# Routing of a mixture-of-experts kernel rewritten: constants ahead of attention, flags on GpSimd, 16-bit one-hot tables, expert 0's weights in batches 1 and 2

## The chip, the cores and the metric

The kernel is one program on one core of a Trainium2 chip. The metric is its device time in microseconds (us), as the median of several executions. The profile and the trace describe one execution. Engines: PE is TensorE, DVE is VectorE, ACT is ScalarE, POOL is GpSimd, SP is SyncE, which here only issues transfers (DMAs).

## The reference

Three stages run one after the other, on 4 batches of 576 positions and 512 channels (8 heads of 64), all in float32:

```python
# 1. windowed attention: heads 0-3 see the last 32 positions, heads 4-7 every 4th of the last 128
attn = softmax(where(mask, q @ k.T / 8, -1e9)) ; x = attn @ v          # (4, 576, 512)
# 2. mixture of 8 experts, one expert for each token
for b in range(B):
    prev_e = -1
    for s in range(S):
        fresh_e = argmax(x[b, s] @ w_gate)
        e = fresh_e if s == 0 or sigmoid(x[b, s] @ w_local) < 0.5 else prev_e
        prev_e = e
        out[b, s] = softmax(x[b, s] @ w_gate)[e] * (relu(x[b, s] @ w1[e]) @ w2[e])
# 3. gated convolution: sigmoid(5-tap causal conv of out) * (out @ w_val), then @ w_out
```

The choice of an expert runs along the sequence: a token either takes its own best expert or keeps the one of the token before it.

## The kernel before, in words

**Attention.** 48 steps (`STEPS` = 12 for each batch: 4 pairs of heads, 3 groups of 2 tiles of 96 queries). In step `s` PE makes the scores of step s, the transposes of s-1, the products with v of s-2 and so on; DVE masks and takes the maximum of s (`mask_and_max`), divides s-2 by its denominator into `x_plain` or `x_dil` (`norm`), and adds up the 9 gate logits of s-5 (`take_logits`). SP's queue, written out by hand, loads `qT`, `kT` and `vwin` ahead of their steps, stores the attention output to `x_tokens` in DRAM, and takes the logits of the dilated heads through DRAM (`dil_logits`, then `lg_back`) to bring them back into token order. Three waits on DVE depend on SP's stores: `norm` of the first step of a batch waits until `x_dil` of the batch before is in DRAM (`dil_stored`), `norm` of its seventh step the same for `x_plain`, and the last `take_logits` of a batch waits for `lg_back` (`lg_loaded`). In the schedule `norm(36)`, the first of batch 3, and the sum of batch 2's logits both stand in the steps that follow step 36.

**Expert weights.** Each expert has four chunks of 128 x 2048. A chunk is loaded twice: by POOL's DMA into `w_high` with rounding (`load_high`), and by SP's into `stage` (`load_raw`, two buffers). POOL then subtracts one from the other into `w_low` (`split`, L564), because every product is made as three passes of rounded parts (`passes`, L1159).

**Routing** is what stands between attention and the first expert tile. DVE takes the largest logit, the best expert, the keep flag (`keep`), and its complement (`anew`). PE transposes `keep` and `start` so that the 96 tokens of a tile lie along a row, DVE scans each row, the ends of the 24 rows are transposed and scanned (`carry`), and the carried choice goes back to [96, 24] (`choice`). `chosen` holds for each token a one-hot row over the experts. Two matmuls (against `before`, a strict triangle, and `ones`) count tokens, DVE works out for each token a slot in the order sorted by expert, each expert's slots starting at a multiple of 128. The slot is split into tile (`hi`) and place (`lo`), one-hot tables `hi_hot`, `hi_tok`, `lo_hot` are made, and 24 matmuls (L1258) invert the map into `token_idx`, by which POOL gathers rows of `x_tokens` (`gather_direct`, `gather_sorted`). `slot_idx` and `batch_tiles` are for the last stage, `prob_slot` scales the experts' output. `link` makes DVE wait for its own last instruction. `keep_clock` issues matmuls of no use so that PE stays busy.

**Experts.** 25 tiles of 128 slots (the last 7 conditional). Each `tile_step` on PE is `up`, the transposes of the next tile, `down` of the tile before, and the transposes of the hidden layer. POOL's `next_expert` loads and splits the next expert when PE has left the buffer. **The last stage** follows, with 18 output tiles.

The order of the work on each engine is that of the code; there is no planner.

## Time and profile before

| | before |
|---|---|
| median of 3 runs | 598.66 us (597.76 to 599.15) |
| the profiled execution's own time | 595.05 us |
| its span, first to last instruction | 593.3 us |
| TensorE busy | 544.3 us (92%) |
| VectorE, ScalarE, GpSimd busy | 267.0, 216.0, 257.3 us |
| mean granted clock of TensorE | 0.965 of full speed |

The profile's page has the engines' busy time, the span in 40 slices, and the chain of work that ended last. The trace behind it can be asked for a stretch of that chain, for the instructions of an engine in order of time with the idle time before each and what ended it, for the transfers with their sizes and times to landing, and for busy time, clock and bytes in any stretch.

### The profile page before, as it was taken

What the parts mean: (1) busy time and instruction counts of PE and PEld (TensorE: products, weight loads), DVE (VectorE), ACT (ScalarE), POOL (GpSimd) and SP (SyncE); (2) the same over time, 40 slices, a digit from 0 to 9 for tenths busy, and PEclk for the clock granted to TensorE, in tenths of its full rate; (3) what the DMA queues carried; (4) which work ended last, traced back from release to release, by engine and by line L of the source; (5) the groups of instructions that cost most, each with busy time, mean ns of one, the idle gap of its engine ahead of it and who ended that gap; (6) DMA issues with size and microseconds to landing.
All of it is one profiled execution on the core that took longest, in us unless ns stands there. A gap on an engine that the chain in (4) does not pass through costs nothing.

```text
span 593.3 us, 10062 instructions
## 1 busy us (share of the span) xinstructions
PE 544.3 (92%) x3274; PEld 461.8 (78%) x3274; DVE 267.0 (45%) x858; ACT 216.0 (36%) x503; POOL 257.3 (43%) x161
## 2 busy tenths in 40 slices
PE   7899999973779999999999999999899586999997
PEld 3789988862568888888888887888688486999986
DVE  4677777755821121312222121122112689998710
ACT  2677777741021221212212121121112555565421
POOL 1000010471168475937275559674953445621210
PEclk9999999995889999999999999999999589999999
DMA  5849499959079996996889797979681522211012
GB/s 170 248 131 265 106 271 315 285 184 288 21 220 372 327 371 210 373 320 244 269 289 312 256 347 221 398 246 382 230 272 51 148 63 66 90 50 54 36 72 88
DMA packets 62772, 128.42 MB, mean 216 GB/s; under 512 B 9664, under 2 KB 17856, under 8 KB 62208
## 3 DMA queue, kind: packets, MB, share of 16 engines
q1 hardware_dynamic: 38560, 68.43, 35.7%
q0 software_dynamic: 17392, 46.93, 24.6%
q10 hardware_dynamic: 6768, 12.36, 6.0%
q8 instruction: 34, 0.56, 0.4%
q14 instruction: 18, 0.15, 0.1%
HBM read 104.28 MB, written 23.41 MB: 215 GB/s over the span
## 4 chain that ended last, share of the span: by engine, by line
PE 56%; DMA 21%; DVE 8%; POOL 6%; issue 5%; SPq 3%; ACT 1%; PEldq 0%; POOLq 0%; ACTq 0%; DVEq 0%
PE bank L1159 39%; DMA stage<-in_moe_w 10%; PE bank L1176 5%; POOL w_low L564 5%; PE bank L1197 4%; DMA w_high<-in_moe_w 3%; DMA dil_logits<-lg_dil 2%; PE bank L1185 2%; PE bank L1312 2%; DVE gate_acc L971 2%; DMA kT<-in_k 2%; DMA stage<-in_moe_w_val 1%; PE bank L1220 1%; DMA vwin<-in_v 1%; PE bank L1375 1%
## 5 line engine op out<-in xcount | busy, mean ns | idle before, releaser
L564 POOL TENSOR_TENSOR w_low<-stage,w_high 128x2048 fp32r<-128x2048 f32 x32 | 146.8, 4595 | 82.3 <-DMA stage<-in_moe_w 59.0
L1159 PE MATMUL bank<-w_high,x_high 128*128 x184 | 74.7, 406 | 5.7 <-POOL w_low L564 3.1
L1014 ACT ACTIVATE probs<-shifted,negmax 96x128 f32<-96x128 f32 x192 | 66.4, 394 | 35.7 <-PE bank L1185 22.1
L1159 PE MATMUL bank<-w_high,h_high 128*128 x184 | 74.2, 403 | 1.4 <-POOL w_low L564 1.4
L917 DVE TENSOR_TENSOR x_low<-bank,x_high 128x512 fp32r<-128x512 f32 x25 | 17.3, 691 | 127.1 <-ACT x_high L1055 127.1
L1159 PE MATMUL bank<-w_high,x_low 128*128 x184 | 72.6, 394 | 0.0
L1159 PE MATMUL bank<-w_low,x_high 128*128 x184 | 72.1, 392 | 0.0
L1159 PE MATMUL bank<-w_high,h_low 128*128 x184 | 72.1, 392 | 0.0
L1159 PE MATMUL bank<-w_low,h_high 128*128 x184 | 71.7, 390 | 0.0
L1055 ACT CAST x_high<-bank 128x512 fp32r<-128x512 f32 x25 | 14.7, 588 | 152.5 <-PE bank L1283 152.5
L553 POOL DMA_DIRECT2D w_high<-in_moe_w x32 | 24.2, 767 | 101.7 <-DVE x_dil L739 83.4
L971 DVE SCALAR_TENSOR_TENSOR gate_acc<-cT,convw,gate_acc 128x576 f32<-128x576 f32 x64 | 64.6, 1028 | 2.3 <-ACT gate_acc L1110 1.7
L1072 ACT CAST h_high<-bank 128x512 fp32r<-128x512 f32 x50 | 26.9, 590 | 105.3 <-PE bank L1312 99.5
L923 DVE TENSOR_SCALAR y_sb<-bank,prob_slot 128x512 f32<-128x512 f32 x25 | 18.8, 750 | 99.6 <-PE bank L1159 99.4
L756 DVE CUSTOM_DVE_ANT_0 shifted<-bank,masks 96x128 f32<-96x128 f32 x192 | 44.1, 283 | 26.2 <-PE bank L1176 26.1
L1176 PE MATMUL bank<-kT,qT 128*96 128x256 f32 x192 | 51.7, 392 | 4.0 <-DMA kT<-in_k 4.0
L685 POOL TENSOR_TENSOR gT_low<-gated,gT_high 128x576 fp32r<-128x576 f32 x16 | 22.8, 1428 | 54.1 <-ACT gT_high L1122 54.1
L1159 PEld LDWEIGHTS bank<-w_high,x_high 128*128 128x128 f32 x184 | 35.0, 190 | 13.2 <-issue 6.6
L1197 PE MATMUL bank<-vwin,probsT 128*96 128x65 f32 x384 | 39.4, 245 | 2.3 <-DMA vwin<-in_v 2.3
L1159 PEld LDWEIGHTS bank<-w_high,h_high 128*128 128x128 f32 x184 | 34.6, 188 | 8.2 <-issue 1.8
L1159 PEld LDWEIGHTS bank<-w_high,x_low 128*128 128x128 f32 x184 | 34.8, 189 | 7.8
L1159 PEld LDWEIGHTS bank<-w_high,h_low 128*128 128x128 f32 x184 | 34.5, 188 | 7.7
(184 smaller groups left out, 1054.5 us busy)
## 6 DMA issues: line engine op xcount, KB each, us to landing
w_high<-in_moe_w POOLq DMA_DIRECT2D x32, 1024.0 KB, 12.8
stage<-in_moe_w SPq DMA_DIRECT2D x32, 1024.0 KB, 7.9
y_sorted<-y_sb ACTq DMA_DIRECT2D x25, 256.0 KB, 7.4
vwin<-in_v SPq DMA_DIRECT2D x4, 1560.0 KB, 7.4
x_sorted<-gathered SPq DMA_DIRECT2D x21, 256.0 KB, 8.2
x_in<-x_sorted ACTq DMA_DIRECT2D x21, 256.0 KB, 5.6
kT<-in_k SPq DMA_DIRECT2D x32, 152.0 KB, 4.7
out<-o_sb SPq DMA_DIRECT2D x18, 256.0 KB, 2.0
```

What stands on the lines that cost most here:

```text
L553: po.dma_start(rows_of(dst, (FF, MODEL)[i]), raw_chunk(e, c)).then_inc(high_loaded[c], 16)
L564: g.tensor_tensor(low, stage[:, c % 2, :], high.bitcast(F32), ALU.subtract).then_inc(split_done, 1)
L685: g.tensor_tensor(gT_low[:, c, at], gated[:, n % 2, :], gT_high[:, c, at].bitcast(F32), ALU.subtract).then_inc(g_split, 1)
L756: d.tensor_tensor_reduce(out=shifted[:, j % 2, u, :], in0=bank[0:QB, j % 2, u * KB:(u + 1) * KB], in1=masks[:, which, :], scale=-SCALE, sc ...
L917: d.tensor_tensor(x_low[:], bank[:, 0, :], x_high[:].bitcast(F32), ALU.subtract).then_inc(xin_split, 1)
L923: d.tensor_scalar(y_sb[:, tile % YB, :], bank[:, 5, :], prob_slot[:, tile:tile + 1], None, ALU.mult).then_inc(y_copied, 1)
L971: d.scalar_tensor_tensor(acc, cT[:, bb % 2, c, which:which + SEQ], convw[:, c, which:which + 1], acc, ALU.mult, ALU.add).then_inc(taps_don ...
L1014: a.activation(probs[:, j % 2, u, :], shifted[:, j % 2, u, :], ACT.Exp, bias=negmax[:, j % 2, u:u + 1], scale=-1.0).then_inc(exp_done, 1)
L1072: a.copy(h_high[:, g * 512:(g + 1) * 512], bank[:, 3 + g, :]).then_inc(hid_high, 1)
L1159: ins = mm(dst, l, r, start=first and i == 0, stop=last and i == 2)
L1176: ins = mm(bank[0:QB, j % 2, w * 2 * KB:(w + 1) * 2 * KB], qT[:, b % 2, n, t * QB:(t + 1) * QB], kT[:, n, :, t * QB:t * QB + KB], start=Tr ...
L1197: ins = mm(bank[0:QB, 4 + j % 2, u * OUTC:(u + 1) * OUTC], probsT[:, j % 2, u * QB:(u + 1) * QB], vwin[:, b % 2, PW * i + u // 2, h, :], s ...
```

## The change

It rewrites the code between attention and the first expert tile, and moves loads:

- The constants (`iota_*`, `ones`, the triangle, now `minus_rest` with -1 in it, and so on) are made by POOL at the program's start, in memory of their own, not after the last store of attention.
- `keep` and `anew` are made by POOL. `keep` is transposed first and alone, ACT copies it to `keep_rows`, and the scans read PSUM directly; several copies from PSUM are gone.
- `chosen` and the running count `upto` are bf16, in the order expert, tile. `upto` is scanned from `chosen` while PE multiplies; PE adds the ranks in PSUM over two matmuls, and a third gives the totals of each batch. What followed for `tile_expert`, `expert_end`, the probabilities and `batch_tiles` stands behind `token_idx` or beside the tables.
- `hi_hot`, `hi_tok`, `hi_prob` and `lo_hot` are made from bf16 inputs, written as pairs of neighbours; `hi_hot` and its kin are 26 wide, not 25; `lo_hot` in two halves, each with its own semaphore.
- SP: chunks 0 and 1 of expert 0 in batch 1, chunks 2 and 3 in batch 2; the fill of the last slots (`y_sorted<-ident`, four DMAs) behind the loads of batch 1's turn, not behind attention. POOL's `load_high(0)` goes with half of batch 1's steps normed, not half of batch 2's; half of expert 1's high weights are asked for ahead of the gathers, the rest behind them.
- PE: 18 `keep_clock` matmuls ahead of the tables, not 30; the expert's number is read ahead of the wait for the first split input.

```diff
@@ sync: load order
-                if b == 2:
+                if b == 1:
                     load_raw(sp, 0, 0)
                     load_raw(sp, 0, 1)
+                if b == 2:
+                    for c in range(2, CHUNKS):
+                        sp.wait_ge(split_done, c - 1)
+                        load_raw(sp, 0, c)
                 store_plain(b)
...
-                if b == 2:
-                    sp.wait_ge(split_done, 1)
-                    load_raw(sp, 0, 2)
-                    sp.wait_ge(split_done, 2)
-                    load_raw(sp, 0, 3)
-
-            for c in range(KD):
-                rows = ys_dram[TOKENS:, c * 128:(c + 1) * 128].rearrange("(t p) c -> p t c", p=128)
-                sp.dma_start(rows, ident[:].unsqueeze(1).broadcast_to([128, ST - TOKENS // 128, 128])
-                             ).then_inc(y_filled, 16)
+                if b == 1:
+                    for c in range(KD):
+                        rows = ys_dram[TOKENS:, c * 128:(c + 1) * 128].rearrange("(t p) c -> p t c", p=128)
+                        sp.dma_start(rows, ident[:].unsqueeze(1).broadcast_to([128, ST - TOKENS // 128, 128])
+                                     ).then_inc(y_filled, 16)
@@ gpsimd
-            po.wait_ge(normed, 2 * STEPS + STEPS // 2)
+            po.wait_ge(normed, STEPS + STEPS // 2)
             load_high(0, 0, 0)
             load_high(0, 0, 1)
             for c in range(CHUNKS):
                 split(0, c, 0)
             po.wait_ge(logits_ready, BATCH)
-            po.wait_ge(plain_stored, 16 * BATCH)
...
+            link(g.tensor_scalar(above[:], logits[:, :, EXPERTS], KEEP_ABOVE, None, ALU.is_gt))
+            g.tensor_tensor(keep[:], above[:], not_first[:], ALU.mult).then_inc(keep_ready, 1)
+            po.wait_ge(keep_ready, 1)
+            g.tensor_scalar(anew[:], keep[:], -1.0, 1.0, ALU.mult, ALU.add).then_inc(anew_ready, 1)
+            po.wait_ge(dil_stored, 16 * len(QUERY_PIECES) * BATCH)
+            load_high(1, 1, 0)
@@ vector: counts and tables
-            link(d.tensor_copy(choice[:], bank[0:QB, 7, 0:TT]))
-            d.tensor_tensor(chosen[:], per_expert(iota_e[:]), per_token(choice[:]), ALU.is_equal
-                            ).then_inc(route_ready, 1)
+            d.tensor_tensor(chosen[:], bank[0:QB, 7, 0:TT].unsqueeze(1).broadcast_to(et), per_expert_t(iota_e[:]),
+                            ALU.is_equal).then_inc(route_ready, 1)
+            dve.wait_ge(route_ready, 5)
+            d.tensor_tensor_scan(upto[:].rearrange("p e t -> p (e t)"), run_on[:].rearrange("p e t -> p (e t)"),
+                                 chosen[:].rearrange("p e t -> p (e t)"), 0.0, ALU.mult, ALU.add
+                                 ).then_inc(route_ready, 1)
...
+            link(d.tensor_tensor(paired(hi_hot[:]), per_tile(iota_hi[:], TT), pairs(hi2[:], SH), ALU.is_equal))
+            d.tensor_tensor(paired(hi_tok[:, :, 0, :]), paired(hi_hot[:]), pairs(iota_t[:], SH), ALU.mult)
+            d.tensor_scalar(hi_tok[:, :, 1, :], hi_hot[:], iota_p[:], None, ALU.mult).then_inc(route_ready, 1)
+            for i in range(HOT_PARTS):
+                part = slice(i * TT // HOT_PARTS, (i + 1) * TT // HOT_PARTS)
+                d.tensor_tensor(paired(lo_hot[:, part, :]), per_tile(iota_lo[:], TT // HOT_PARTS),
+                                pairs(lo2[:, part, :], 128), ALU.is_equal).then_inc(lo_ready, 1)
@@ tensor
-            keep_clock(w_high[:, 0, :], 30, 5)
-            pe.wait_ge(route_ready, 6)
+            keep_clock(w_high[:, 0, :], 18, 5)
+            pe.wait_ge(route_ready, 7)
             for t in range(TT):
-                ins = mm(bank[:, 6, 0:2 * ST], lo_hot[:, t, :], hi_tok[:, t, :, :].rearrange("p a s -> p (a s)"),
+                if t % (TT // HOT_PARTS) == 0:
+                    pe.wait_ge(lo_ready, t // (TT // HOT_PARTS) + 1)
+                ins = mm(bank[:, 3, 0:2 * SH], lo_hot[:, t, :], hi_tok[:, t, :, :].rearrange("p a s -> p (a s)"),
                          start=t == 0, stop=t == TT - 1)
             ins.then_inc(route_mm, 1)
             keep_clock(w_high[:, 0, :], 12, 5)
-            pe.wait_ge(token_ready, 1)
+            pe.wait_ge(experts_ready, 1)
...
             def up(s):
+                e = expert_of(s)
                 pe.wait_ge(xin_split, s + 1)
-                e = expert_of(s)
```

On SP's queue, the first place is where batch 1's turn ends and batch 2's begins (`vwin` is the load for batch 3, `x_dil` and `dil_logits` are stores of batch 2). Before:

```order
L397 DMA qT<-in_q 128x576 [waits scores_done]
L402 DMA kT<-in_k 64x608 x2
L407 DMA vwin<-in_v 128x3120 [waits pv_done]
L414 DMA x_tokens<-x_dil 192x1x256 [waits normed]
L414 DMA x_tokens<-x_dil 96x1x256 x2
L414 DMA x_tokens<-x_dil 192x1x256
L420 DMA dil_logits<-lg_dil 192x1x9 [waits lg_taken]
```

With the change, in the same place:

```order
L409 DMA qT<-in_q 128x576 [waits scores_done]
L414 DMA kT<-in_k 64x608 x2
L419 DMA vwin<-in_v 128x3120 [waits pv_done]
L475 DMA y_sorted<-ident 128x7x128 x4
L426 DMA x_tokens<-x_dil 192x1x256 [waits normed]
L426 DMA x_tokens<-x_dil 96x1x256 x2
L426 DMA x_tokens<-x_dil 192x1x256
L432 DMA dil_logits<-lg_dil 192x1x9 [waits lg_taken]
```

The four fills now stand ahead of batch 2's stores. Further up in the same turn stand the two `stage` loads that stood in batch 2's.

On DVE's queue, the second place is the slots and the tables. Before, from the slot to `token_idx`:

```order
L871 CAST slot_i<-slot 96x24
L873 TENSOR_SCALAR lo_i<-slot_i 96x24 [waits dve_chain]
L874 TENSOR_SCALAR hi_i<-slot_i 96x24
L875 CAST lo<-lo_i 96x24 [waits dve_chain]
L876 CAST hi<-hi_i 96x24
L877 TENSOR_TENSOR hi_hot<-iota_s,hi 96x600 [waits dve_chain]
L879 TENSOR_TENSOR hi_tok<-hi_hot,iota_t 96x24x25 [waits dve_chain]
L880 TENSOR_SCALAR hi_tok<-hi_hot,iota_p 96x24x25
L881 TENSOR_TENSOR lo_hot<-iota_lo,lo 96x3072
L884 SCALAR_TENSOR_TENSOR reach<-tstart,upto 96x32
...
L892 COPY tok_parts<-bank 128x50 [waits route_mm]
L893 SCALAR_TENSOR_TENSOR token_idx<-tok_parts 128x25 [waits dve_chain]
```

With the change:

```order
L882 CAST slot_i<-slot 96x24 [waits dve_chain]
L883 TENSOR_SCALAR hi_i<-slot_i 96x24 [waits dve_chain]
L884 TENSOR_SCALAR lo_i<-slot_i 96x24
L885 CAST hi_113<-hi_i 96x48 [waits dve_chain]
L886 CAST lo_114<-lo_i 96x48
L897 TENSOR_TENSOR hi_hot<-iota_hi,hi_113 96x624 [waits dve_chain]
L898 TENSOR_TENSOR hi_tok<-hi_hot,iota_t 96x24x26 [waits dve_chain]
L899 TENSOR_SCALAR hi_tok<-hi_hot,iota_p 96x24x26
L902 TENSOR_TENSOR lo_hot<-iota_lo,lo_114 96x1536 x2
L905 CAST expert_end<-tend 96x8
L906 TENSOR_TENSOR ended<-iota_s,tend 96x200
L909 COPY tok_rest<-bank 128x25 [waits route_mm,dve_chain]
```

The number of instructions is the same up to `lo_hot`; the forms are 16-bit, and behind `lo_hot` stand two short ones where five stood.

On PE's queue, the third place is the start of the first `up`. Before, and with the change:

```order
L1283 MATMUL bank<-ident,x_in 128x128 [waits token_ready,xin_direct0]
L1283 MATMUL bank<-ident,x_in 128x128 x3
L1270 TENSOR_LOAD tile_expert [waits xin_split]
L1270 ISA x2
L1301 ISA
L1159 ISA [waits split_done]
```

```order
L1337 MATMUL bank<-ident,x_in 128x128 [waits experts_ready,xin_direct0]
L1337 MATMUL bank<-ident,x_in 128x128 x3
L1324 TENSOR_LOAD tile_expert
L1324 ISA x2
L1355 ISA [waits xin_split]
L1205 ISA [waits split_done]
```

The read of `tile_expert` now stands ahead of the wait for `xin_split`.

## Rows read from the trace of the kernel before

**Rows 1.** The page: busy us, share of the span, instructions.

```profile
PE 544.3 (92%) x3274; PEld 461.8 (78%) x3274; DVE 267.0 (45%) x858; ACT 216.0 (36%) x503; POOL 257.3 (43%) x161
```

**Rows 2.** The chain that ended last, 88:200 us: start, us, what.

```profile
102.35 0.34 SPq L425
...
108.66 9.34 DMA kT<-in_k
...
129.96 5.75 DMA x_tokens<-x_plain
...
138.17 0.36 DVE top L806
...
158.68 0.20 DVE token_idx L893
...
159.73 3.27 DMA x_in<-x_tokens,token_idx
...
165.12 1.17 issue
...
166.29 7.09 PE bank L1159 x24
...
188.93 5.49 PE bank L1159 x24
```

**Rows 3.** The waits of PE, 166:470 us: total us, times, longest.

```profile
PE bank L1159 <- POOL w_low L564: 4.5, 3, 3.0
```

**Rows 4.** The timeline of DVE and PE in attention: start, us, instruction, idle before.

```profile
77.42 0.21 DVE L780 TENSOR_TENSOR logits<-lg_plain,lg_back 96x54 f32<-96x54 f32 x1
...
102.88 0.42 DVE L739 TENSOR_TENSOR x_dil<-bank,rden 96x256 f32<-96x256 f32 x1
...
105.78 0.21 DVE L780 TENSOR_TENSOR logits<-lg_plain,lg_back 96x54 f32<-96x54 f32 x1
...
118.04 1.10 PE L1176 MATMUL bank<-kT,qT 128*96 128x256 f32 x4 [1.05 <-DMA kT<-in_k]
...
132.42 0.21 DVE L780 TENSOR_TENSOR logits<-lg_plain,lg_back 96x54 f32<-96x54 f32 x1 [1.78 <-DMA lg_back<-dil_logits]
```

**Rows 5.** The transfers: issuing engine, count, size of one, median us to landing.

```profile
stage<-in_moe_w SPq DMA_DIRECT2D x32, 1024.0 KB, 7.9
vwin<-in_v SPq DMA_DIRECT2D x4, 1560.0 KB, 7.4
kT<-in_k SPq DMA_DIRECT2D x32, 152.0 KB, 4.7
qT<-in_q SPq DMA_DIRECT2D x15, 288.0 KB, 4.8
x_tokens<-x_plain SPq DMA_DIRECT2D x4, 576.0 KB, 5.4
y_sorted<-ident SPq DMA_DIRECT2D x4, 448.0 KB, 5.9
lg_back<-dil_logits SPq DMA_DIRECT2D x4, 20.2 KB, 3.0
```

**Rows 6.** The timeline of DVE in the routing.

```profile
144.32 0.35 DVE L835 TENSOR_TENSOR chosen<-iota_e,choice 96x192 f32<-96x192 f32 x1
...
147.34 0.30 DVE L852 TENSOR_TENSOR over<-upto,tile_mult 96x144 f32<-96x144 f32 x1
...
151.40 0.17 DVE L871 CAST slot_i<-slot 96x24 int32<-96x24 f32 x1
...
152.19 0.78 DVE L877 TENSOR_TENSOR hi_hot<-iota_s,hi 96x600 f32<-96x600 f32 x1
...
153.70 0.52 DVE L880 TENSOR_SCALAR hi_tok<-hi_hot,iota_p 96x600 bf16<-96x600 f32 x1
...
154.14 3.35 DVE L881 TENSOR_TENSOR lo_hot<-iota_lo,lo 96x3072 bf16<-96x3072 f32 x1
```

**Rows 7.** One us of the windows: us, PE, PEld, DVE, ACT, POOL busy, PEclk, DMA share, GB/s.

```profile
166.00:167.00 1.00, 0.71 (x2) 0.62 (x3) 0.00 (x0) 0.00 (x0) 0.70 (x2) 0.50 0.62 213
```

More of the change, by code:

```diff
@@ L152, in build @@
         cand = table("cand", te, F32)
-        cand2 = table("cand2", te, F32)
         fresh = table("fresh", [QB, TT], F32)
+        above = table("above", [QB, TT], F32)
         keep = table("keep", [QB, TT], F32)
@@ L201, in build @@
-        reach_tiles = fixed("reach_tiles", [QB, EXPERTS, BATCH], I32)
+        tend = hots("tend", [QB, EXPERTS], F32)
+        tstart = hots("tstart", [QB, EXPERTS], F32)
+        slot_i = hots("slot_i", [QB, TT], I32)
+        tok_rest = hots("tok_rest", [128, ST], F32)
+        ended = hots("ended", [QB, ST, EXPERTS], F32)
+        tile_e = hots("tile_e", [QB, ST], F32)
+        reach = hots("reach", [QB, EXPERTS, BATCH], F32)
+        so_far = hots("so_far", [QB, EXPERTS, BATCH], F32)
+        reach_used = hots("reach_used", [QB, EXPERTS, BATCH], F32)
@@ new lines, in _ @@
+            link(d.reduce_sum(ntiles[:], over[:], AX.X))
+            link(d.tensor_tensor_scan(tend[:], ones_e[:], ntiles[:], 0.0, ALU.mult, ALU.add))
+            link(d.tensor_tensor(tstart[:], tend[:], ntiles[:], ALU.subtract))
+            link(d.scalar_tensor_tensor(sums[:], per_expert_t(tstart[:]), 128.0,
+                                        bank[0:QB, 6, 0:TT * EXPERTS].rearrange("p (e t) -> p e t", e=EXPERTS),
+                                        ALU.mult, ALU.add))
+            link(d.tensor_tensor(sums2[:], sums[:], chosen[:], ALU.mult))
@@ new lines, in _ @@
+            dve.wait_ge(route_mm, 6)
+            link(d.tensor_copy(tok_rest[:], bank[:, 3, SH:SH + ST]))
+            d.scalar_tensor_tensor(token_idx[:], bank[:, 3, 0:ST], float(QB), tok_rest[:],
+                                   ALU.mult, ALU.add).then_inc(token_ready, 1)
+            link(d.reduce_sum(tile_e[:], ended[:], AX.X))
+            d.tensor_scalar(tile_expert[:], tile_e[:], float(EXPERTS - 1), None, ALU.min).then_inc(experts_ready, 1)
+            link(d.tensor_tensor(picked[:], expd[:], chosen[:].rearrange("p e t -> p t e"), ALU.mult))
@@ L851, in _ @@
-            most = TOKENS // 128
-            link(d.tensor_tensor(over[:], upto[:, :, TT - 1:TT].broadcast_to([QB, EXPERTS, most]),
-                                 tile_mult[:].unsqueeze(1).broadcast_to([QB, EXPERTS, most]), ALU.is_gt))
-            link(d.reduce_sum(ntiles[:], over[:], AX.X))
-            link(d.tensor_tensor_scan(tend[:], ones[:, 0:EXPERTS], ntiles[:], 0.0, ALU.mult, ALU.add))
-            d.tensor_copy(expert_end[:], tend[:])
-            d.tensor_tensor(ended[:], iota_s[:].unsqueeze(2).broadcast_to([QB, ST, EXPERTS]),
-                            tend[:].unsqueeze(1).broadcast_to([QB, ST, EXPERTS]), ALU.is_ge)
@@ L905, in sum_probs, with weight_hots @@
+            def weight_hots():
+                for i in range(3):
+                    d.tensor_tensor(paired(hi_prob[:, :, i, :]), paired(hi_hot[:]), pairs(prob_parts[:, i], SH), ALU.mult
+                                    ).then_inc(parts_ready, 1)
             def sum_probs():
```

287 lines of the change are left out of this document (148 added, 139 removed).

## The prediction

> **What bounds the kernel now.** I read the page first: PE is busy for 92% of the span [rows 1], so a gain must come from places where PE does nothing useful. The chain that ended last shows where [rows 2]. Up to 130 us it runs through attention and SP's transfers. From 138.17 to 158.68 it stays on DVE, with short visits to PE: the routing, some 20.7 us. Then a gather takes 3.27 us, the first `up` starts at 166.29, and from there the chain is PE's tiles. The waits of PE between 166 and 470 us come to 4.5 us on split weights in 3 pieces [rows 3]. So after 166.29 everything hangs on PE's start; the weight pipeline takes its own start from buffers that PE frees, and moves with it. The change is worth what it moves the first `up`, with one more place to look at: attention, since the loads moved into it use SP's queue.
>
> In the timeline of attention [rows 4] the same sum of logits stands at 77.42 and 105.78, so one batch takes 28.36 us. At 118.04 PE waited 1.05 us for `kT`. At 132.42 DVE had waited 1.78 us for `lg_back`: without that the logits would have been summed from 130.64 on.
>
> **Term 1, the start of the routing.** Before, `top` started at 138.17, held by the constants, which POOL made only after the last store of `x_plain` (129.96 + 5.75) had landed [rows 2]. After, the constants are long there. SP no longer waits for split chunks ahead of batch 3's stores, so `lg_back` is in time. So `logits` follows the last sum at 130.64 + 0.05, takes 0.21 [rows 4], and `top` starts at 130.93: **7.24 us earlier**, if attention ends when it did. `x_plain` still has to be in DRAM before the gather, some 12 us later, so its 5.75 us are covered; without that cover they would stand in front of the gather. POOL's constants now lie beside the first loads of attention, at no cost.
>
> **Term 2, attention with more on SP's queue.** In batch 1's turn the queue gets what it had in batch 2's: one pair's `qT` and two `kT`, 288 + 2 x 152 = 592 KB, two `stage` chunks (2048), `x_plain` (576), another pair (592) [rows 5], together 3808 KB. Before, that ran from 102.7 (after the 0.34 us issue at 102.35) to 108.66 + 9.34 = 118.0 [rows 2]. A transfer of 20 KB (`lg_back`) took 3.0 us to land [rows 5]; I take these 3.0 as fixed, and get 3808 / (15.3 - 3.0) = 310 KB per us. The rival reading, nothing fixed, gives 249.
>
> Shifted by one batch, the piece runs from 74.3 to 89.6, and PE's stall of 1.05 us now comes in batch 1. Behind it stand, in SP's order, two more pairs (1184), `vwin` (1560), the four fills (1792), and only then `x_dil` of batch 2 (576, as `x_plain`): 8920 KB in all. At 310 it lands at 74.3 + 28.8 + 3.0 = 106.1. `norm(36)` waits for just this store before it overwrites `x_dil`; before, it ran at 102.88 [rows 4], now it is due at 103.9. Stall: 2.2 us. The logits' stores go behind it, with 1 us for their many small pieces (my estimate), land at 107.1, and `lg_back` is there 0.34 + 3.0 later, at 110.4; the sum that needs it is due at 105.78 + 1.05 + 2.2 = 109.0. Stall: 1.4. The pair for the last steps then follows as before, 118.0 - 102.35 = 15.65 us behind the logits' landing, at 122.8, due at 117.0 + 1.05 + 3.6 = 121.6. Stall: 1.2. Together 1.05 + 2.2 + 1.4 + 1.2 = 5.85 us, against 1.05 before: **4.8 us later**. Behind DVE, queued on its own engine, the masks of the next steps wait in each of these stalls, and so do ACT and PE. Bounds: at 249 KB per us `x_dil` lands at 110.1 and the loss is 8.8 us (6.2 + 1.4 + 1.2); above 354 (8920 / 25.2) nothing stalls but the 1.05, and the loss is 0. I take 4.8.
>
> **Term 3, the routing itself**, by DVE's timeline [rows 6], from `top` (before: 20.7 us to the end of `token_idx`). An instruction of 192 elements takes 0.35 us, with 0.03 to 0.04 between linked ones.
> - To the end of `chosen`: 144.67 - 138.17 = 6.5 before. Out go one 192-element add (0.38), `keep` and `anew` (0.4, to POOL), one transpose (0.2), a copy before and a scan between (0.7), two short copies (0.4). The copies that ACT takes over lie beside DVE's scans. Some 2 us; I have **2.0**. POOL's three small instructions have 1.5 us, in which DVE does four; if they took longer, `start` would wait.
> - `chosen` to `over`: 2.67 before, in which two f32 matmuls, a copy and a scan followed each other. Now the scan (192 elements, 0.55 at most 0.6) lies beside the first matmul, the rest is bf16: about 1.1. **1.6**.
> - `over` to `slot_i`: 151.40 - 147.34 = 4.06. Now `over`, `ntiles`, `tend`, `tstart`, `sums`, `sums2`, `slot`: 0.34 + 0.33 + 0.21 + 0.19 + 3 x 0.38 = 2.2. **1.8**.
> - `slot_i` to `hi_hot`: 0.79 before, five short ones as before: 0.
> - `hi_hot` to the end of `lo_hot`: 157.49 - 152.19 = 5.3. The trace has no all-16-bit two-input instruction. Bounds: one element per cycle as in `lo_hot` (3072 in 3.35 us) and `hi_hot` (600 in 0.78) gives no gain at 5.3; two elements per cycle, as the one-input row shows (600 in 0.52, with about 0.15 fixed), gives 0.50 + 0.40 + 0.24 + 1.83 = 2.97, a gain of 2.3. I take the fast end: DVE does reach two per cycle in this stage, and both the inputs and the layout in pairs are what halves the words it reads. **2.3**.
> - behind `lo_hot`: 1.38 before (five short instructions, then two). Now PE's second half of 12 matmuls beside two instructions, then two: 0.95. **0.4**.
>
> Sum **8.1 us**; it would be 5.8 with the slow end.
>
> The Trainium skill, "VectorE: DVE Perf Modes", section "The perf-mode tier table", says that `tensor_tensor` on bf16 in SBUF runs at two elements per cycle and on fp32 at one. The f32 half agrees with the 3.35 us of `lo_hot` (0.92 elements per ns) [rows 6]; the bf16 half no row here shows.
>
> **Term 4, from `token_idx` to the first `up`.** Before 7.4 us, of which 1.17 stand as issue between `x_low` and the first matmul [rows 2]: the read of `tile_expert` behind the wait. Now it is read during the split: **1.1 us** less. The probabilities, moved ahead of the first `low_x`, take some 4.6 us behind `token_idx` and have 5.5; if DVE were a microsecond slower it would show. The gather is new company: two `stage` chunks and two `w_high` chunks, 4096 KB, are asked for within 1 us of `top`. At 310 KB per us they land 13.2 + 3.0 = 16 us after it; the gather is issued at about 13.4 and is due at 16.7. Bounds 0 and 3 us; I take **1.0 us** lost, since nearly all of them are through by then.
>
> The Trainium skill, "DMA: Bandwidth & Descriptors", section "Issuing engines are not separate DMA queues", says that transfers issued from different engines run on the same 16 DMA engines. By that the gather would share with all four chunks, which is the upper bound's case, and moving loads to another queue would gain nothing.
>
> **Clock.** The first `up` took 7.09 us, a later one 5.49 [rows 2]; the granted clock was 0.50 at 166 us, the level of 1.2 GHz [rows 7], after PE had stood idle but for four transposes. PE's idle stretch becomes shorter by 1.1 us, and of the 18 + 12 spacers the last ones end earlier. I leave it as it was; if the clock held, 1.6 us more would come.
>
> **Sum.** 7.24 - 4.8 + 8.1 + 1.1 - 1.0 = 10.6 us. The profiled execution took 595.05 us with a span of 593.3, so it would take about 584.4. The median of the three runs is 3.6 us above that execution; from it, 598.66 - 10.6 = 588.0.
>
> **Rivals.**
> 1. *No new stall in attention* (0.24). For it: 354 KB per us is only 14% above my rate, and the fills are plain. Against it: the `kT` of 118.0 was late with 3808 KB, and here 8920 stand ahead. Time: 588.0 - 4.8 = 583.2.
> 2. *The 16-bit tables stay at one element per cycle* (0.12): broadcast operands might keep DVE from it. 590.3.
> 3. *Slower than before* (0.04): attention becomes bound by SP's queue. The gain is gone when `x_dil` of batch 2 lands at 116.8 or later, which takes a rate below 8920 / 39.5 = 226 KB per us. The fills are the suspect, with 128-element pieces; the lowest rate I can read, 249, gives 592.0. Time: 600 or more.
> 4. *The rest is late in another way* (0.12): the gather behind the weights by the full 3 us, or a short stall at 77 us, where `lg_back` was just in time, or the clock falling in a stall of attention. About 591.
>
> My forecast has the rest, 0.48. Less than 0.2% is about what a measurement of this kernel cannot tell from no change: 0.02. Slower 0.05, faster 0.93.
>
> **Range.** Low: rival 1 with the clock held, 583.2 - 1.6 = 581.6. High: the slow rate and the slow tables, 588.0 + 4.0 + 2.3 = 594.3. I give 581.5 to 594.
>
> **What would show it.** `top` would start near 135.8 with term 2, near 131 without. DVE would wait for the stores of `x_dil` near 104 us and for `lg_back` near 109, PE for `kT` near 88.6 and 121.6. `top` to the end of `token_idx` would take 12.6 us, `lo_hot` 0.95 us for each half, `token_idx` to the first `up` 7.3. The waits for split weights after the first `up` would still be near 4.5 us. The prediction is wrong if the tiles start on time and are then held by expert 1's weights, or if attention's stalls exceed 9 us.

## The result and the profile after

The changed kernel takes 592.44 us (median of 20 runs, 587.64 to 600.9) against 597.56 us (median of 20, 593.3 to 605.57) for the kernel before. The ratio is 0.9925, with a 95% interval of 0.990 to 0.995: about 4.5 us faster, where 10.6 were forecast. The profiled execution took 590.49 us with a span of 588.7, against 595.05 and 593.3 before: 4.6 us. The ratios here and below leave out executions in a slower state (the medians of all 20 differ by 5.1 us), and where the profiled execution was such a one, only waits and durations inside it are read, not its span.

The chain of the changed kernel that ended last, from 60 to 166 us (start, us, what; steps of PE in attention left out):

```profile
80.33 10.58 DMA kT<-in_k
...
114.91 9.67 DMA kT<-in_k
...
149.73 1.75 DVE lo_hot L902 x2
...
152.59 0.80 issue
153.39 3.46 DMA x_in<-x_tokens,token_idx
...
159.27 6.91 PE bank L1205 x23
```

The first `up` starts at 159.27, not at 166.29 [rows 2]: 7.0 us earlier. The timeline of DVE and PE (start, us, instruction, idle before) has the steps on the way:

```profile
77.51 0.21 DVE L806 TENSOR_TENSOR logits<-lg_plain,lg_back 96x54 f32<-96x54 f32 x1
...
90.96 2.02 PE L1222 MATMUL bank<-kT,qT 128*96 128x256 f32 x4 [2.23 <-DMA kT<-in_k]
...
107.01 0.42 DVE L765 TENSOR_TENSOR x_dil<-bank,rden 96x256 f32<-96x256 f32 x1 [0.25 <-DMA x_tokens<-x_dil]
...
111.57 0.21 DVE L806 TENSOR_TENSOR logits<-lg_plain,lg_back 96x54 f32<-96x54 f32 x1 [1.91 <-DMA lg_back<-dil_logits]
...
124.62 1.90 PE L1222 MATMUL bank<-kT,qT 128*96 128x256 f32 x4 [2.33 <-DMA kT<-in_k]
...
139.37 0.35 DVE L835 TENSOR_REDUCE top<-logits 96x24 f32<-96x192 f32 x1
...
146.97 0.62 DVE L881 TENSOR_REDUCE slot<-sums 96x24 f32<-96x192 f32 x1
...
152.33 0.19 DVE L910 SCALAR_TENSOR_TENSOR token_idx<-bank,tok_rest 128x25 uint32<-128x25 f32 x1
```

`top` was due at 135.8 by the prediction and starts at 139.37. Up to 77.5 us the two traces agree within 0.1 us [rows 4], so all of it is lost between there and 139. The windows of the changed kernel (us, then PE, PEld, DVE, ACT, POOL busy, PEclk, DMA share, GB/s) show two things in it:

```profile
78.00:82.00 4.00, 4.00 (x42) 3.66 (x40) 3.27 (x24) 3.22 (x11) 0.00 (x0) 1.00 0.99 330
...
86.00:90.00 4.00, 2.73 (x28) 2.40 (x26) 2.56 (x16) 3.08 (x11) 4.00 (x2) 1.00 1.06 304
...
92.00:94.00 2.00, 2.00 (x11) 1.66 (x10) 0.93 (x8) 0.59 (x2) 0.63 (x1) 0.50 1.14 297
...
94.00:98.00 4.00, 4.00 (x38) 3.61 (x38) 2.60 (x16) 2.91 (x11) 0.00 (x0) 0.99 0.94 342
...
126.00:128.00 2.00, 2.00 (x13) 1.80 (x12) 0.93 (x8) 1.05 (x4) 0.12 (x1) 0.50 0.00 0
```

From 78 to 102 us the DMA engines have a busy share of 0.94 to 1.12. That alone does not make a wait: the kernel before has 0.82 to 1.48 in the same stretch, and PE waits for no `kT` there. One of its windows:

```profile
98.00:102.00 4.00, 4.00 (x38) 3.54 (x37) 2.89 (x20) 2.98 (x11) 0.00 (x0) 1.00 1.48 334
```

What differs is what stands ahead of the `kT` in SP's queue. And behind each wait of PE for `kT` the granted clock stands at 0.50, the level of 1.2 GHz, for 3.4 us: the four `scores` matmuls at 90.96 take 2.02 us where the full clock gives 1.10 [rows 4]. SP's timeline shows where its queue stood:

```profile
85.72 14.71 SPq L475 DMA_DIRECT2D y_sorted<-ident  x4
100.47 4.00 SPq L426 DMA_DIRECT2D x_tokens<-x_dil  x4
104.53 2.54 SPq L432 DMA_DIRECT2D dil_logits<-lg_dil  x4
108.39 0.34 SPq L437 DMA_DIRECT2D lg_back<-dil_logits  x1
```

The four issues of the fills take 14.71 us, and the stores of `x_dil` and of the logits stand behind them. SP can ask for batch 3's `kT` only when the logits are through, so the fills reach the second wait for `kT` by that way.

### The profile page after: what moved, and what is told of

The parts are those of the page before. It is cut to its first block, busy times and chain, and to the rows that moved or that the text cites. A ratio compares the mean times of both kernels' runs of the same rounds, so it can differ in the third digit from the quotient of the medians.

```text
span 588.7 us, 10040 instructions
## 1 busy us (share of the span) xinstructions
PE 547.1 (93%) x3261; PEld 464.1 (79%) x3261; DVE 261.9 (44%) x851; ACT 216.5 (37%) x505; POOL 258.4 (44%) x167
## 4 chain that ended last, share of the span: by engine, by line
PE 74%; DMA 10%; DVE 6%; issue 4%; SPq 2%; POOL 2%; ACT 1%; another core or an unknown queue 1%; PEldq 0%; POOLq 0%; DVEq 0%; ACTq 0%
PE bank L1205 53%; PE bank L1222 6%; PE bank L1243 4%; DMA kT<-in_k 3%; PE bank L1366 3%; DMA stage<-in_moe_w 2%; PE bank L1231 2%; POOL w_low L608 2%; DVE gate_acc L1013 2%; DMA w_high<-in_moe_w 2%; PE bank L1337 2%; PE bank L1429 1%; PE bank L1266 1%; DMA vwin<-in_v 1%; PE bank L1255 1%
## 5 line engine op out<-in xcount | busy, mean ns | idle before, releaser
L1222 PE MATMUL bank<-kT,qT 128*96 128x256 f32 x192 | 53.4, 403 | 7.7 <-DMA kT<-in_k 7.7
L1205 PEld LDWEIGHTS bank<-w_high,x_high 128*128 128x128 f32 x184 | 35.2, 192 | 12.3 <-issue 5.6
L1205 PE MATMUL bank<-cT_high,wv_high 128*128 128x288 f32 x128 | 41.3, 322 | 0.0
L1205 PEld LDWEIGHTS bank<-w_low,x_high 128*128 128x128 f32 x184 | 35.4, 192 | 6.6
```

Source lines behind the costliest of these rows:

```text
L1205: ins = mm(dst, l, r, start=first and i == 0, stop=last and i == 2)
L1222: ins = mm(bank[0:QB, j % 2, w * 2 * KB:(w + 1) * 2 * KB], qT[:, b % 2, n, t * QB:(t + 1) * QB], kT[:, n, :, t * QB:t * QB + KB], start=Tr ...
```

## The experiments

Each ran against the kernel before on the same chip (its medians there: 597.55, 595.28, 599.98 and 597.04 us in the four sets).

**Apart: the loads alone, the routing alone.** `loads_only` is the kernel before with the change's order of the loads; `routing_only` is the changed kernel with the order of before.

```diff
 # loads_only, in the kernel before (routing_only: the reverse, in the changed kernel)
-                if b == 2:
+                if b == 1:
                     load_raw(sp, 0, 0)
                     load_raw(sp, 0, 1)
...
+                if b == 1:
+                    for c in range(KD):          # the fills of y_sorted
...
-            po.wait_ge(normed, 2 * STEPS + STEPS // 2)
+            po.wait_ge(normed, STEPS + STEPS // 2)
```

> The kernel before with only the loads moved: SP's weight loads of expert 0 in batches 1 and 2, the four fills in batch 1's turn, POOL's load of expert 0 half a batch after batch 1 began. The routing is the old one. Theory (queue): attention ends some 8 us later, as with the whole change (its last sum of logits stood at 138.95 us, before at 130.64), with PE waiting over 2 us for kT near 89 and again near 122 us, and the granted clock at 0.5 behind each; the fills, which stood before the constants' last wait, no longer delay anything, so the kernel is 6 to 8 us slower than before: ratio 1.010 to 1.014. Rival (downstream): attention's stalls cost little and the change's gain was lost behind the first expert tile; then this kernel is within 0.3% of the one before.

> The changed kernel with the loads of attention put back where they stood before: weights of expert 0 in batch 2, the four fills behind attention. Theory (queue): attention ends as before, the last sum of logits at about 130.6 us and logits at 132.4, because lg_back is late again by 1.8 us; top starts at 132.7, 5.5 us earlier than before, routing 7.5 us and the way to the first up 0.7 us shorter as in the changed kernel's trace: 13.7 us less, ratio about 0.977, and better than the whole change by 8 to 9 us. Rival (downstream): the first up starts 13 us earlier, but the time falls by no more than the whole change's 4.5 us, ratio 0.99 or above.

Measured: `loads_only` 602.33 us, ratio 1.0155 (1.007 to 1.024); `routing_only` 585.73 us, ratio 0.985 (0.976 to 0.994). So the loads in their new order are a loss by themselves (1.010 to 1.014 was expected), and the routing alone brings more than the whole change by its ratio, though the intervals overlap. In `loads_only` SP's timeline has the same hold, and DVE's waits (total, times, longest) what follows from them:

```profile
89.00 14.70 SPq L463 DMA_DIRECT2D y_sorted<-ident  x4
```

```profile
DVE logits L779 <- DMA lg_back<-dil_logits: 5.4, 2, 3.9
DVE x_dil L738 <- DMA x_tokens<-x_dil: 1.0, 1, 1.0
```

`routing_only` pays at another place. PE's waits between 145 and 165 us:

```profile
PE bank L1338 <- DMA x_in<-x_tokens,token_idx: 4.8, 1, 4.8
```

The changed kernel waits 2.1 us there: with the fills behind attention, the gather takes 6.17 us instead of 3.46, with the DMA engines at 1.03 or more until 156 us. That is 2.7 us of what it missed 0.977 by. The rest was lost earlier: its `top` stands at 137.63, not at 132.7. The sum of batch 1's logits is 4.2 us later than before (81.58 against 77.42), with the clock at 0.50 from 17.6 to 24.6 us, and a wait of 1.83 us for `kT` in batch 3 is followed by 3.4 us at 0.50.

**Where the fills stand.** Three kernels keep everything of the change but the place of the fills: in batch 0's turn (`fill_b0`), behind attention (`fill_end`), and in the expert phase behind the third group of sorted tiles, with ACT's wait for them moved to its tile 18 (`fill_mid`).

```diff
-                if b == 1:
-                    for c in range(KD):          # the fills
...
+                if b == 0:                       # fill_b0
...
+            for c in range(KD):                  # fill_end: behind the loop over the batches
...
             store_sorted(2)
+            for c in range(KD):                  # fill_mid
```

> The changed kernel with only the four fills moved from batch 1's turn on SP's queue to batch 0's, where the DMA engines moved 146 GB/s. Theory (fills): SP is no longer held for 14.7 us behind the fills; x_dil and the logits of batch 2 are stored 10 us earlier, so the wait for lg_back and the second wait for kT (2.33 us) with its stretch at the low clock go: attention ends 4 to 5 us earlier than in the changed kernel, top near 134.5. The first wait for kT near 89 us (2.2 us and its clock) stays near 1 to 2 us, since the weights still stand ahead of it. Ratio 0.983 to 0.986. Rival (weights): the two weight chunks make all of the stalls, the fills none; then the ratio stays at 0.992 and both waits for kT stay above 2 us.

> The changed kernel with only the four fills moved back behind attention, ahead of expert 1's first stage load. Theory (fills): as with the fills in batch 0, top near 134.5; the gather then stands behind 1792 KB more and may come up to 2 us later. Ratio 0.983 to 0.989. Rival (weights): 0.992, both waits for kT above 2 us.

> The changed kernel, with the four fills of y_sorted asked for only behind the third group of sorted tiles, in the expert phase; ACT waits for them before it stores tile 16, not at its start. Theory (the fills hold SP's queue in batch 1, which starves the kT loads and drops TensorE's clock; put behind attention they delay the gather, put in the expert phase they disturb nothing): top near 131.4, as with the fills right behind attention, the gather no later than in the changed kernel (first up 6.7 us behind token_idx, so near 151.5), no wait for y_filled; the median 3 to 5 us below fill_end's ratio of 0.986, so 0.977 to 0.982. Rival (the two stage and two w_high chunks of expert 0 are what makes attention late and gather late, the fills are harmless): top stays near 139 and the ratio near 0.9925.

Measured: `fill_b0` 591.26 us, 0.9917 (0.987 to 0.996), where 0.983 to 0.986 was expected; `fill_end` 584.72, 0.9861 (0.976 to 0.996); `fill_mid` 585.24, 0.981 (0.973 to 0.989). `fill_end` has `top` at 131.39 with no stall but 1.2 us for `kT`, and then the wait of 4.8 us for `x_in`, as `routing_only`. In `fill_b0` the stall has only moved to batch 1, as DVE's and PE's waits show:

```profile
DVE x_dil L765 <- DMA x_tokens<-x_dil: 7.1, 1, 7.1
```

```profile
PE bank L1255 <- DVE lg_plain L802: 5.7, 1, 5.7
```

In `fill_mid` the timeline of SP, PE and DVE has these rows, and `top` starts 5.7 us earlier than in the changed kernel:

```profile
88.97 2.53 SPq L426 DMA_DIRECT2D x_tokens<-x_dil  x4
...
92.30 1.10 PE L1222 MATMUL bank<-kT,qT 128*96 128x256 f32 x4 [1.40 <-DMA kT<-in_k]
...
95.36 2.83 SPq L432 DMA_DIRECT2D dil_logits<-lg_dil  x4
...
133.68 0.35 DVE L834 TENSOR_REDUCE top<-logits 96x24 f32<-96x192 f32 x1
```

The stores of `x_dil` are issued 11.5 us earlier; one wait of 1.40 us for `kT` is left, and the four matmuls behind it take 1.10 us: the clock did not fall. 133.7 is 2.3 us later than expected; this execution lost that ahead of 76 us, where its `lg_back` stands 2.1 us later (75.90, against 73.81), with the clock at 0.50 from 19 to 23 us. The gather was not late: first `up` at 153.44, 6.6 us behind `token_idx`. The fills in batch 1 cost the changed kernel about 1.1% (0.981 against 0.9925, whose intervals just part; against its second measurement below, 0.9869, taken in the same set as `fill_mid`, it is 0.6%, and there the intervals overlap).

Single traces do not settle it, so here is the same stretch in all of them, from the start of batch 1's sum of logits to that of the last sum. With the fills in batch 1 it takes 61.5 (the changed kernel), 67.5 (`after_again`), 62.9 (`after_spacers`), 67.1 (`fill_wide`), 65.3 (`tables_f32`) and 62.1 us (`loads_only`). With the fills elsewhere it takes 53.7 to 55.7 us in seven traces, the kernel before among them with 55.0 (`fill_b0` loses its time ahead of this stretch), and 62.5 in one, `fill_mid_late_high`, whose attention is coded as that of `fill_mid`. There the first wait for `kT` was followed by 13.7 us at the lower clock, with no fill near (PE's timeline and windows):

```profile
90.40 2.02 PE L1221 MATMUL bank<-kT,qT 128*96 128x256 f32 x4 [2.16 <-DMA kT<-in_k]
```

```profile
96.00:100.00 4.00, 4.00 (x22) 3.52 (x21) 1.85 (x12) 1.97 (x6) 0.00 (x0) 0.50 0.88 306
```

The two waits have two sources. The `kT` of the first takes 9.5 to 12.3 us from issue to landing in the six traces with the fills behind it, and 9.9 to 10.8 in four without them (`fill_b0`, `fill_end`, `fill_mid`, `fill_mid_late_high`): the fills do not make it late. The wait for batch 3's `kT` stands in all six with the fills in batch 1 (0.51 us of it behind spacers, otherwise 0.94 to 2.80) and in none of these four.

**The weights.** `fill_mid_weights_b2` also puts expert 0's chunks back in batch 2. `fill_mid_late_high` asks for expert 1's first `w_high` chunks behind the gathers again.

```diff
 # fill_mid_weights_b2, against fill_mid
-                if b == 1:
+                if b == 2:
                     load_raw(sp, 0, 0)
                     load_raw(sp, 0, 1)
...
 # fill_mid_late_high, against fill_mid
-            po.wait_ge(dil_stored, 16 * len(QUERY_PIECES) * BATCH)
-            load_high(1, 1, 0)
...
             gather_direct(3)
+            load_high(1, 1, 0)
             load_high(1, 1, 1)
```

> As fill_mid, and expert 0's weights are loaded in batch 2 again, as before the change. It parts the moved weights from the moved fills. If the weights in batch 1 cost attention anything, top comes earlier than in fill_mid (by up to 1.2 us, the wait for kT in batch 1); against that the split waits and the traffic of batch 3's loads come back: top within 1 us of fill_mid's, the two last chunks' splits nearer to the first up, ratio within 0.004 of fill_mid. If the weights were the cause of the 8.3 us lost in attention, top would be 4 us or more earlier than in fill_mid.

> As fill_mid, and POOL asks for expert 1's first two w_high chunks only behind the gathers, where the kernel before had them. Theory A (the gather shares the 16 DMA engines with these two chunks): PE's wait for x_in falls from about 2.1 to about 0.9 us, first up about 1.2 us earlier, and the price is a longer wait for expert 1's split weights (w_low) in the first tiles, some 1 to 2 us: ratio within 0.002 of fill_mid. Theory B (the gather is late by its own latency of 3.3 to 3.5 us, the chunks do nothing): the wait for x_in stays near 2.1 us.

Measured: `fill_mid_weights_b2` 583.18 us, 0.9801 (0.974 to 0.986): its `top` at 134.14 is within 0.5 us of `fill_mid`'s. The weights in batch 1 neither cost nor bring anything that can be seen in the total: the wait for `kT` moves with them, 1.40 us in batch 2 against 1.10 in batch 3 here, where DVE also waits 1.83 us for `lg_back`. `fill_mid_late_high` 591.84 us, 0.9914 (0.987 to 0.996). PE's waits from 150 to 440 us:

```profile
PE bank L1204 <- POOL w_low L607: 9.0, 4, 4.9
PE bank L1336 <- DMA x_in<-x_tokens,token_idx: 2.2, 1, 2.2
```

In `fill_mid` the wait for `x_in` was 2.0 us: theory B holds, the two chunks do not delay the gather. The waits for split weights are 7.4 us longer than the 1.6 of `fill_mid`, where I had expected 1 to 2. But `fill_mid_weights_b2`, which asks for the chunks early, has 7.2 us of them too, so that sum alone does not show what the late chunks cost; the ratio is 1.0% above `fill_mid`'s, with intervals that overlap. Nor can the ratio be put on the chunks: with the same code, attention took 8.8 us longer in this trace than in `fill_mid`'s. What late chunks cost stays open.

**The changed kernel once more**, for a second trace.

> The changed kernel itself, once more, for a second trace of it. Theory (the lengths of attention's stalls come from the order of the queue and repeat; the stretch at the lower clock in the last stage falls at another place in each execution): top at 139.4 within 0.5, first up at 159.3 within 0.7, the two waits for kT above 2 us in the same places, but the stretch of 1.2 GHz behind 470 us elsewhere or shorter. Rival (that stretch comes from the change): it stands at 493 to 500 again with the wait ahead of it. Ratio 0.990 to 0.995.

Measured: 588.66 us, ratio 0.9869 (0.980 to 0.994). The fills hold SP's queue for 13.54 us, and the waits for `kT` are there again, but `top` stands at 146.75, 7.4 us later, where 0.5 was allowed, and the ratio is below the 0.990 to 0.995 expected. Of the five traces of this order with the new routing, the first has the earliest `top` (139.37; the others 144.38 to 147.53). The timeline and the windows of PE:

```profile
92.32 1.10 PE L1222 MATMUL bank<-kT,qT 128*96 128x256 f32 x4 [2.15 <-DMA kT<-in_k]
...
128.14 2.02 PE L1222 MATMUL bank<-kT,qT 128*96 128x256 f32 x4 [2.39 <-DMA kT<-in_k]
```

```profile
130.00:134.00 4.00, 4.00 (x22) 3.63 (x21) 1.84 (x12) 1.97 (x6) 0.41 (x1) 0.50 0.00 1
...
138.00:141.00 3.00, 3.00 (x16) 2.52 (x16) 0.93 (x8) 1.35 (x5) 0.00 (x0) 0.50 0.13 7
```

The same waits are followed by 6.8 and 13.7 us at 1.2 GHz, instead of 3.4 and 3.4. A microsecond at that level costs half a microsecond where PE is the bound. Of the 7.4 us, 1.4 were lost ahead of the first wait (92.32 against 90.96), 2.2 between the two (3.4 us more at the low level give 1.7), and 3.9 behind the second (10.3 us more give up to 5.2).

**Spacers in the wait.** Nine matmuls that nobody reads are put right before the two waits.

```diff
+                if j >= 2:
+                    pe.wait_ge(shifted_done, UNITS * (j - 1))
+                if j in (2 * STEPS + 9, 3 * STEPS + 9):
+                    keep_clock(warm, 9, j % 2)
                 if i == 0:
                     pe.wait_ge(qk_loaded[b % 2][n], 48 * (b // 2 + 1))
-                if j >= 2:
-                    pe.wait_ge(shifted_done, UNITS * (j - 1))
```

> The changed kernel with 9 spacer matmuls of 128x512 (bf16, of the resting pattern that the kernel has elsewhere) on PE right before each of the two waits for kT in batches 2 and 3, some 1.9 us each at full clock. Theory (the waits of 2.2 us let TensorE's clock fall to 1.2 GHz, and the stretch behind them, 3.5 to 14 us long in the traces of the changed kernel, costs half its length): the waits shrink below 0.6 us, the granted clock stays at 1.0 behind 91 and 124 us, top starts at 136 to 137 instead of 139.4 to 146.8, and the ratio is 0.983 to 0.989. Rival (the clock falls for another reason than the idle stretch, as it does at 18 us, or the spacers draw it down themselves): the low stretches stand where they stood and top stays at 139 or later.

Measured: 594.55 us, ratio 0.9874 (0.982 to 0.993). The first wait was a long one in this execution, and 3.23 us of it were left behind the spacers: the clock fell, from 98 to 105 us. At the second, 0.51 us were left:

```profile
128.96 1.89 PE L1212 MATMUL bank<-warm 128*128 128x512 bf16 x8
131.36 1.10 PE L1224 MATMUL bank<-kT,qT 128*96 128x256 f32 x4 [0.51 <-DMA kT<-in_k]
```

```profile
128.00:132.00 4.00, 3.42 (x23) 2.06 (x23) 1.27 (x10) 1.75 (x6) 4.00 (x2) 1.00 0.86 264
132.00:136.00 4.00, 4.00 (x42) 3.64 (x41) 2.84 (x21) 2.60 (x9) 2.03 (x1) 1.00 0.04 5
```

and the clock stayed at 1.00. That is what the theory says of the place where the spacers did fill the wait, in one trace; that the clock would have fallen there without them is likely by the other traces, not shown. `top` at 144.38 did not come earlier (136 to 137 was expected), and the ratio cannot be told from the other kernels with the fills in batch 1.

**The size of the pieces.** The same fill with pieces of 1024 bytes instead of 512 (the filler rows hold zeros).

```diff
-                    for c in range(KD):
-                        rows = ys_dram[TOKENS:, c * 128:(c + 1) * 128].rearrange("(t p) c -> p t c", p=128)
...
+                    wide = warm[:].bitcast(F32)
+                    for c in range(MODEL // 256):
+                        rows = ys_dram[TOKENS:, c * 256:(c + 1) * 256].rearrange("(t p) c -> p t c", p=128)
+                        for t in (slice(0, 4), slice(4, 7)):
```

> The changed kernel with the same fill at the same place in SP's queue, the same bytes in the same count of four transfers, but cut in pieces of 1024 bytes from a [128, 256] tile instead of 512 bytes from ident (the filler rows hold zeros instead of ident). Theory A (it is the number of small pieces that holds SP's queue for 14.7 us): SP's time for the four issues falls to about half, 7 to 8 us, the stores of x_dil of batch 2 go out 6 us earlier, the logits' return and the kT for the last steps are in time, top near 135. Theory B (it is the bytes ahead of them in the queue, 6712 KB at some 250 to 310 KB per us, that hold it): SP stays held for 12 us or more and top stays near 139.

Measured: 593.58 us, ratio 0.9871 (0.982 to 0.992). SP's timeline:

```profile
89.21 4.84 SPq L478 DMA_DIRECT2D y_sorted<-warm  x4
94.09 13.07 SPq L426 DMA_DIRECT2D x_tokens<-x_dil  x4
107.22 2.54 SPq L432 DMA_DIRECT2D dil_logits<-lg_dil  x4
```

The issues of the fills take a third, and those of `x_dil` behind them take what is missing: 17.9 us for the eight, against 18.7. `top` stands at 147.53, with waits of 2.09 and 2.80 us for `kT`. Theory A is refuted: with half the pieces the hold is as long and only falls on other issues, as theory B has it. (Ahead of the fills stand 6552 KB by the prediction's own sizes, not 6712.) I had read the 14.71 us as a property of the fills; the issue that comes next takes it, whichever it is.

**The tables in f32.** The numbers that are compared are f32 again, the tables bf16.

```diff
-        iota_hi = kept("iota_hi", [QB, SH], BF16)
-        iota_lo = kept("iota_lo", [QB, 128], BF16)
+        iota_hi = kept("iota_hi", [QB, SH], F32)
+        iota_lo = kept("iota_lo", [QB, 128], F32)
...
-        lo2 = table("lo2", [QB, TT, 2], BF16)
+        lo2 = table("lo2", [QB, TT, 2], F32)
```

> The changed kernel with the counts and the slot numbers that feed the one-hot tables in f32 again (iota_hi, iota_lo, hi2, lo2), all else kept. If the two-input instruction runs at two elements per cycle because all its operands are 16-bit, hi_hot goes back from 0.48 to about 0.8 us and the two halves of lo_hot from 1.82 to about 3.4 us, while hi_tok (still bf16 in and out) stays at 0.48: the end of token_idx is 1.9 us later behind top, 15.0 instead of 13.1. Rival (it is the layout in pairs or the bf16 output alone): they stay at 0.48 and 1.82.

Measured: 593.15 us, ratio 0.9897 (0.986 to 0.994). DVE's timeline, of it and then of `after_spacers`, which has the tables as the change makes them:

```profile
154.21 0.81 DVE L897 TENSOR_TENSOR hi_hot<-iota_hi,hi 96x624 bf16<-96x624 f32 x1
...
155.75 3.42 DVE L902 TENSOR_TENSOR lo_hot<-iota_lo,lo 96x1536 bf16<-96x1536 f32 x2
```

```profile
153.44 0.48 DVE L897 TENSOR_TENSOR hi_hot<-iota_hi,hi 96x624 bf16<-96x624 bf16 x1
...
154.64 1.82 DVE L902 TENSOR_TENSOR lo_hot<-iota_lo,lo 96x1536 bf16<-96x1536 bf16 x2
```

With everything else kept, layout too, 16-bit inputs take about half the time: 0.48 for 0.81, 1.82 for 3.42. That refutes the expectation's rival, the layout or the output alone. `top` to the end of `token_idx` takes 15.05 us (145.16 to 160.21) against 13.15.

**The order within the queue.** `fill_mid` with the two chunks behind `vwin`.

```diff
-                if b == 1:
-                    load_raw(sp, 0, 0)
-                    load_raw(sp, 0, 1)
                 store_plain(b)
...
                     load_v(b + 2)
+                if b == 1:
+                    load_raw(sp, 0, 0)
+                    load_raw(sp, 0, 1)
```

> As fill_mid, and the two stage chunks of expert 0 stand at the end of batch 1's turn in SP's queue, behind the pairs and vwin, no longer ahead of x_plain and of the kT that PE waits for. Theory (it is the 2624 KB ahead of that kT, two chunks and x_plain, that make it late; what stands behind it only stretches it): PE's wait of 1.4 us for kT in batch 2 goes, kT lands within 6 to 7 us of its issue instead of 10.3, no low stretch of the clock in batch 2 or 3, top 1 to 2 us earlier than in fill_mid as counted from the first logits, ratio 0.976 to 0.982. Rival (the 16 DMA engines are shared by whatever is asked for, in front or behind): kT still takes 9 us or more and the wait stays above 1 us; the chunks behind vwin may then make the store of x_dil of batch 2 late instead, with a wait of DVE of 1 us or more near 103 us.

Measured: 587.02 us, ratio 0.978 (0.972 to 0.984). PE's wait in batch 2 is gone: between 60 and 100 us it waits for nothing. In batch 3, where the other two chunks and `x_plain` still stand ahead of the `kT` (10.26 us from issue to landing), the wait is back, and the clock falls again (timeline, then windows):

```profile
121.20 2.01 PE L1222 MATMUL bank<-kT,qT 128*96 128x256 f32 x4 [2.04 <-DMA kT<-in_k]
```

```profile
122.00:124.00 2.00, 2.00 (x10) 1.52 (x10) 0.75 (x7) 0.36 (x2) 0.43 (x1) 0.50 0.12 39
```

From batch 1's sum of logits to `top` it took 56.0 us, against 54.0 in `fill_mid`, where 1 to 2 us less was expected. This kernel, `fill_mid` and `fill_mid_weights_b2` (0.978, 0.981, 0.980) cannot be told from each other; each beats the one before, and each beats the changed kernel's 0.9925. Against its 0.9869 the intervals overlap.

## Why the prediction was right or wrong

The direction and the place of the loss were right. The size was not, 10.6 us forecast and 4.5 measured, and one part of the mechanism, the clock, stood in a rival and not in the sum. By the terms, in the pair of profiled executions:

- **Term 1**: right. `top` follows the last sum of logits (ended at 138.95) by 0.42 us; 0.29 was forecast.
- **Term 2** is the step that failed. It priced attention's stalls at 4.8 us over before; that sum ended 8.3 us later (130.64 before, 138.95 after), near the bound of 8.8. The route from the queue was right (`kT` twice, `lg_back`; DVE's wait for the store of `x_dil` was 0.25, not 2.2). The failure has two parts. The waits for `kT`: 2.23 and 2.33 us, 4.6 instead of the 1.05 + 1.2 that I had. I had carried the `kT` of batch 1's turn over with its old transfer time, but it was issued at 80.33 and took 10.58 us, not 9.34 [rows 2]. Two chunks and `x_plain` stand ahead of it; without the chunks there (`fill_mid_stage_last`) PE does not wait, without the fills behind it the transfer is as long. Why it took 1.2 us more than the same piece took a batch later before is open. And the clock: the prediction put its fall in attention at nothing, and named it only in rival 4. Behind the waits stand 3.4 + 3.4 us at 1.2 GHz, 3.4 us lost. With 3.5 us more wait for `kT` than before (4.56 - 1.05) that makes 6.9 of the 8.3; the rest I have not split (DVE waits 1.91 us for `lg_back` and 0.25 for `x_dil`). That the stall of 2.2 us at `x_dil` did not come hid part of the error. Rival 4's 591 was nearest; rival 1, no new stall, is refuted.
- **Term 3**: 7.6 of 8.1 us (20.71 to 13.15). `lo_hot` took 0.91 us for each half, against 0.95. Of the half microsecond missing, `slot` is half: 0.62 us over a strided view of 192 elements, where I had 0.38. Rival 2 falls: the Trainium skill, "VectorE: DVE Perf Modes", "The perf-mode tier table", gives `tensor_tensor` on bf16 in SBUF two elements per cycle, and `tables_f32` agrees (0.48 against 0.81 us, 1.82 against 3.42).
- **Term 4**: better than forecast. `token_idx` to the first `up` is 6.75 us, not 7.3. The issue gap fell from 1.17 to 0.31 us, and the gather took 3.46 instead of 3.27: 0.2 lost, not 1.0. The upper bound of 3 us did not come: `fill_mid_late_high` moves two chunks away and the wait stays at 2.2. In the changed kernel the DMA share is down to 0.14 from 152 to 154 us, where the gather starts: the chunks had landed. In `fill_end` it is 1.02 or more until 150 us, and the gather issued at 145.42 takes 6.17 us. The Trainium skill, "DMA: Bandwidth & Descriptors", "Issuing engines are not separate DMA queues", says that transfers of all issuing engines run on the same 16 DMA engines; `fill_end` agrees, and the other two traces had nothing left to share with.
- **Behind the first `up`**, where the prediction had no term: 7.0 us of gain at 159.27 are 4.6 at the end. In the last stage the chain of the changed kernel has the first of the rows below, and that of the kernel before the second:

```profile
495.00 8.41 PE bank L1205 x36
```

```profile
501.93 6.00 PE bank L1159 x36
```

The same 36 matmuls take 2.41 us more. The windows of the changed kernel around them:

```profile
492.00:494.00 2.00, 0.52 (x4) 0.36 (x4) 2.00 (x5) 0.45 (x1) 1.15 (x1) 0.86 0.14 25
494.00:496.00 2.00, 1.87 (x9) 1.90 (x10) 1.98 (x4) 1.21 (x3) 0.00 (x0) 0.50 0.22 74
```

The clock is at 1.2 GHz from 493.4 to 500.2. In `after_again` the stretch near there is 3.4 us long, not 6.8, and `loads_only`, with the old routing, has one of 3.4 us too. From the first `up` to the end nine traces have anything from 422 us (`routing_only`) to 429 us (the changed kernel): this part differs from execution to execution. Whether the change makes it more likely is open.

Together: of the 10.6 us, term 2 took 3.5, terms 1 and 3 took 0.7, term 4 gave 0.6 back, and 2.4 went in the last stage. That this pair gives 4.6, as the ratio does, is partly chance: in the other five traces with the fills in batch 1 attention took longer still.

The fills in batch 1, then, cost some 0.6 to 1.1% of the 1.9% that the change brings without them in attention; 6 to 14 us more in attention in six traces show the loss more clearly than the ratios do. That they are the suspect stood in rival 3, with their small pieces as the reason; the pieces are not it.

## What to carry to other kernels

When loads are moved earlier, add up the bytes that stand ahead of each transfer that an engine will wait for, in the order of the issuing queue, and do so for the stores too: a queue that is held issues the next load later. A high DMA share is no sign by itself, the kernel before had it without a wait. Price a new wait of TensorE not by its length alone: 2 us of waiting cost another 1.7 to 6.8 us by the lower clock here, and which it is differs between executions of one kernel. So compare several traces before putting microseconds on one edit. Work that nobody waits for, such as a fill, belongs where the DMA share is low, and neither in the middle of a paced loop nor right in front of a gather.

## What the runs showed of the hardware

- The clock after a wait for `kT` in attention. Waits of 1.05 (before), 1.40 (`fill_mid`) and, behind spacers, 0.51 us were followed by a granted clock of 1.00; waits of 1.8 to 3.2 us in eight traces were all followed by 0.50. The stretches were 3.4, 6.8 or 13.7 us long, and which of them followed was not fixed by the wait: 2.33 us gave 3.4, and 2.39 us gave 13.7. It is not a clean rule: in `loads_only` 1.43 us were enough, in `fill_b0` 1.52 us were not, and at the start of attention waits of 2.2 to 2.3 us for `vwin` were left without a fall in the traces before and after.
- SP's issues of a `qT` or `kT` take 0.5 to 0.6 us where little is under way. The four fills took 14.71 us in the changed kernel and 3.6 to 5.6 us in the expert phase of the kernels with `fill_mid` in their name; the hold passes to whatever stands next (13.07 us for the four of `x_dil` in `fill_wide`).
- A reduction over a strided view of 192 elements took 0.62 us, where one over the plain layout takes 0.35 (`top`).
